# Three float32 layers on one core: the first three tiles' steps written out anew, a second output bank for two tiles, other weight addresses

## What is computed

```python
for t in range(S):      # S = 768, 8 heads of width 64
    state = gamma * state + outer(k[t], v[t])
    x[t] = q[t] @ state / sqrt(64)
h = x @ w_in            # 512 -> 1024
e = exp(h - max(h)); sm = e / (sum(e) + 1e-9); solu = h * sm
ln = (solu - mean(solu)) / sqrt(var(solu) + 1e-6) * g_ln
x = ln @ w_out          # 1024 -> 512
h = x @ w_in2           # 512 -> 2048
y = (h * cos(h)) @ w_out2
```

## Time and profile before

| | us |
|---|---|
| median of 3 runs (958.66 to 959.32) | 958.75 |
| the profiled execution | 958.3 |
| its span | 956.5 |
| PE busy | 931.4 |
| DVE busy | 732.5 |
| ACT busy | 563.0 |
| POOL busy | 265.3 |

### The profile page before, as it was taken

The page is one execution under the profiler, slowest core; times in us unless marked ns, Lnnn a source line. Parts: engine busy times, 40 slices in busy tenths (PEclk is TensorE's granted clock), DMA queues, the critical chain, the costliest instruction groups (busy, mean ns, idle before and its releaser), DMA issues.

```text
span 956.5 us, 14711 instructions
## 1 busy us (share of the span) xinstructions
PE 931.4 (97%) x4992; PEld 826.1 (86%) x4992; DVE 732.5 (77%) x1054; ACT 563.0 (59%) x923; POOL 265.3 (28%) x260
## 2 busy tenths in 40 slices
...
DMA packets 106520, 148.18 MB, mean 155 GB/s; under 512 B 7408, under 2 KB 77040, under 8 KB 106480
## 3 DMA queue, kind: packets, MB, share of 16 engines
...
...
## 4 chain that ended last, share of the span: by engine, by line
PE 81%; DVE 12%; issue 4%; ACT 1%; DMA 1%; POOL 0%; DVEq 0%; SPq 0%; ACTq 0%; POOLq 0%
PE bank L318 26%; PE bank L321 26%; PE bank L320 26%; DVE p_l L1111 2%; DVE q_l L1095 1%; PE bank L620 1%; DVE work L1161 1%; DVE p_m L1104 1%; DVE x_l L1135 1%; DVE nmax L1155 1%; DVE wo_out L1209 1%; PE bank L655 1%; DVE z_l L1189 1%; ACT x_h L788 1%; DVE work L1201 1%
## 5 line engine op out<-in xcount | busy, mean ns | idle before, releaser
L321 PE MATMUL bank<-yc_h,ring 128*128 128x384 f32 x448 | 150.6, 336 | 0.0
L320 PE MATMUL bank<-yc_l,ring 128*128 128x384 f32 x448 | 150.5, 336 | 0.0
L318 PE MATMUL bank<-yc_h,ring 128*128 128x384 f32 x448 | 150.3, 336 | 0.0
L1238 DVE SCALAR_TENSOR_TENSOR gg<-turns,c 128x768 f32<-128x768 int32 x64 | 61.1, 954 | 63.8 <-ACT turns L859 63.8
L1035 POOL TENSOR_TENSOR y_raw<-y_raw,t 128x768 f32<-128x768 f32 x4 | 7.4, 1851 | 362.0 <-DVE yc_l L1220 362.0
L865 ACT ACTIVATE gg<-gg 128x768 f32<-128x768 f32 x64 | 54.2, 847 | 81.0 <-DVE gg L1245 80.9
L859 ACT ACTIVATE turns<-c 128x768 int32<-128x768 f32 x64 | 54.2, 847 | 80.5 <-DVE c L1308 78.0
L318 PEld LDWEIGHTS bank<-yc_h,ring 128*128 128x128 f32 x448 | 84.2, 188 | 8.3 <-issue 0.4
L320 PEld LDWEIGHTS bank<-yc_l,ring 128*128 128x128 f32 x448 | 84.1, 188 | 8.1
L321 PEld LDWEIGHTS bank<-yc_h,ring 128*128 128x128 f32 x448 | 84.1, 188 | 0.0
L318 PE MATMUL bank<-w1i_h,x_h 128*128 128x512 f32 x192 | 78.5, 409 | 5.0 <-DVE x_l L1135 3.6
...
## 6 DMA issues: line engine op xcount, KB each, us to landing
ring<-w_split SPq DMA_DIRECT2D x224, 256.0 KB, 2.8
...
```

The lines of the kernel that those rows point to most:

```text
L318: eng.matmul(dst, ah, bh, start=first and i == 0, stop=False, skip_group_check=read_between)
L320: eng.matmul(dst, ah, bl, start=False, stop=False, skip_group_check=read_between)
L321: m = eng.matmul(dst, al, bh, start=False, stop=last_one and i == n - 1, skip_group_check=read_between)
L1238: dve.scalar_tensor_tensor(gg[:, r, :], turns[:, r, :], -TWO_PI_HI, flat(c_32[:, r, :, :]), ALU.mult, ALU.add)\
```

## The change

- `head` is written out anew. The steps of the first three tiles stand in one explicit list, and `STEP` holds from n = 3 on. Among what moves: on tile 0, PL and ST stand ahead of PK of tile 1, O1 directly behind O0; SC of tile 1 and W1 2 and 3 stand ahead of L1a of tile 0; PK of tile 2 stands behind EX and U of tile 0. W1 0 to 3 stay in front of L1a; W1 4 stands behind SL of tile 1, and units 5, 6 and 7 stand behind SC, T0 and T1 in n = 3 (`between`), so 4 to 7 all come later than before.
- DVE's `nmax` gets a step name of its own, NM. In `STEP` it stands behind L1b, where it was; in the explicit list behind ST of tile 1.
- `bank_o`: O1 of tiles 0 and 1 writes the bank `ps_t`, so it doesn't wait for `x_l` of O0. T0 of tile 0, which writes that bank next, gets a wait for the last `x_l` of tile 1.
- q of tile 0 is scaled by DVE instead of POOL (`q_sc0`), and for the first two tiles DVE starts on the first half of `q_h` (`q_hi0`) before ACT has made the second.
- The memsets are split: four in front (`zeros(0)`), four in DVE's PK of tile 1 (`zeros(1)`), with the semaphore `q_zero` for SC. PE starts on `ld_cst` instead of `setup`.
- Loads: q of tile 0 goes first, then the constants, then k; k and q of tile 1 stand ahead of the first W1 unit.
- `ident` is read where it lies in the constants, so its copy and its tile go. With that and other fillers, `w1i`, `x` and `work` lie 320 bytes higher, `z`, `w1o` 192 bytes lower, `w2o` 576 bytes lower. Within 512 bytes the start of `w1i_h` goes from 224 to 32 and that of `w2o` from 0 to 448.

```diff
-        ("DL", 1), ("T1", 3), ("EX", 2), ("ST", 1), ("WS", 0),
+        ("NM", 2), ("DL", 1), ("T1", 3), ("EX", 2), ("ST", 1), ("WS", 0),
...
-            sb1("to_64_bytes", [128, 4])
+            sb1("to_512_bytes", [128, 84])
-            ident = sb1("ident", [128, 128])
-            sb3("to_w2o", [128, 656])
+            sb3("to_w2o", [128, 512])
+        ident = cst[:, ID0:QSC0]
...
-        early = {(1, "PL"): (0,), (1, "PQ"): (1,), (1, "O1"): (2, 3),
-                 (2, "O0"): (4,), (2, "PN"): (5,), (2, "CEN"): (6, 7)}
...
+        head += [("PK", 0), ("PQ", 0), ("PV", 0), ("PN", 0)]
+        head += [("SC", 0), ("DL", 0), ("PL", 0), ("ST", 0), ("PK", 1), ("O0", 0), ("O1", 0),
+                 ("PQ", 1), ("W1", 0), ("SH", 0), ("PV", 1), ("W1", 1), ("PN", 1), ("SL", 0)]
+        head += [("SC", 1), ("W1", 2), ("W1", 3), ("L1a", 0), ("L1b", 0), ("DL", 1), ("PL", 1),
+                 ("ST", 1), ("NM", 0), ("EX", 0), ("U", 0), ("PK", 2), ("O0", 1), ("O1", 1),
+                 ("SH", 1), ("PQ", 2), ("PV", 2), ("SQ", 0), ("CEN", 0), ("PN", 2), ("VAR", 0),
+                 ("SL", 1), ("W1", 4)]
+        between = {(3, "SC"): 5, (3, "T0"): 6, (3, "T1"): 7}
+        for n in range(3, TILES):
+            for name, behind in STEP:
                 head += [(name, n - behind)] * (n >= behind)
+                if (n, name) in between:
+                    head.append(("W1", between[n, name]))
...
+        def bank_o(t, b, g):
+
+            return ps_t if g == 1 and by_dve(t, b) else ps_o
...
+            sp.dma_start(raw[:, 0, 0, :], qT[0, :, :]).then_inc(ld_kq[0], 16)
             sp.dma_start(cst[:, 0:MASK0], consts[:, 0:MASK0]).then_inc(ld_cst, 16)
-            load_kq(0, 0)
+            sp.dma_start(raw[:, 0, 1, :], kT[0, :, :]).then_inc(ld_kq[0], 16)
...
+            load_kq(1, 1)
             load_w1(0)
-            load_kq(1, 1)
...
                     wait(pe, k_lo, b, t)
+                    if by_dve(t, b):
+                        pe.wait_ge(q_zero, t + 1)
...
-                    wait(pe, xl_done, b, t, 2, g - 1)
+                    if by_dve(t, b):
+                        wait(pe, xl_done, b, t - 1, 2, g)
+                    else:
+                        wait(pe, xl_done, b, t, 2, g - 1)
...
+                        if isinstance(b, int) and t == 0:
+                            wait(pe, xl_done, b, FIRST - 1, 2, 1)
...
-            pe.wait_ge(setup, SETUP)
+            pe.wait_ge(ld_cst, 16)
...
                 if name == "PK" and by_dve(t, b):
+                    if t == 1:
+                        zeros(1)
+                    if t == 0:
+                        q = raw[:, par, 0, :]
+                        loaded(dve, ld_kq, t, b)
+                        dve.tensor_tensor(q, q, qsc, ALU.mult).then_inc(q_sc0, 1)
                     wait(dve, k_hi, b, t)
...
-                    wait(dve, q_hi, b, t)
                     if by_dve(t, b):
+                        wait(dve, q_hi0, b, t)
...
-                elif name == "L1b":
+                elif name == "NM":
                     wait(dve, l1_done, b, t, 2, 1)
```

More of the change, by code:

```diff
@@ L46 @@
 TS = SUPER // 128
-QSC0 = 0
+ID0 = 0
+QSC0 = ID0 + 128
 KSC0 = QSC0 + PAIRS * C
 GC0 = KSC0 + H
-ID0 = GC0 + PAIRS
-MASK0 = ID0 + 128
+MASK0 = GC0 + PAIRS
 NCONST = MASK0 + H * C
@@ L61 @@
 W1_SLOTS = 4
-SETUP = 6
 FIRST = 2
@@ L184, in build @@
         ksc = cst[:, KSC0:GC0]
-        gam_c = cst[:, GC0:ID0]
+        gam_c = cst[:, GC0:MASK0]
+        ident = cst[:, ID0:QSC0]
         e_b, u_b, c_b = work[:, 0, :], work[:, 1, :], work[:, 2, :]
@@ L195, in build @@
         ld_w1 = [sem(f"ld_w1_{u}") for u in range(W1_UNITS)]
-        setup = sem("setup")
+        setup, q_zero = sem("setup"), sem("q_zero")
         w1_hi, w1_lo = sem("w1_hi"), sem("w1_lo")
-        q_sc, n_sc = sem("q_sc"), sem("n_sc")
+        q_sc0, q_sc, n_sc = sem("q_sc0"), sem("q_sc"), sem("n_sc")
+        q_hi0 = sem("q_hi0")
         k_hi, q_hi, n_hi, v_hi = sem("k_hi"), sem("q_hi"), sem("n_hi"), sem("v_hi")
@@ L256, in build @@
         head, tail = [], []
-        for n in range(TILES):
-            first = []
-            if n == 0:
-                first = [("PK", 0), ("PQ", 0), ("PV", 0), ("PN", 0)]
-            elif n == 1:
-                first = [("SC", 1), ("PK", 0), ("PL", 1), ("DL", 1), ("ST", 1), ("O0", 1), ("PV", 0),
-                         ("PQ", 0)]
-            elif n == 2:
-                first = [("PK", 0), ("PV", 0), ("SC", 1)]
-            steps = first + [part for part in STEP if part not in first]
-            for name, behind in steps:
+        head += [("PK", 0), ("PQ", 0), ("PV", 0), ("PN", 0)]
[8 more added lines that the diff above has]
+            for name, behind in STEP:
                 head += [(name, n - behind)] * (n >= behind)
-                head += [("W1", u) for u in early.get((n, name), ())]
+                if (n, name) in between:
+                    head.append(("W1", between[n, name]))
         body = [(name, n - behind) for n in range(TILES) for name, behind in STEP]
@@ L276, in build @@
         tail += [("L1a", last), ("T0", last - 1), ("YH", P6), ("YL", P6), ("YH", P5), ("L1b", last),
-                 ("T1", last - 1), ("EX", last), ("P", P1), ("TBL", 0), ("LA", last - 1),
+                 ("NM", last), ("T1", last - 1), ("EX", last), ("P", P1), ("TBL", 0), ("LA", last - 1),
                  ("U", last), ("CEN", last), ("P", P2), ("SQ", last), ("LB", last - 1),
@@ L590, in step @@
                                           q_of(q_h, par, p), q_of(q_l, par, p)))
-                        m = products(pe, ps_o[:, o], terms, True, True)
+                        m = products(pe, bank_o(t, b, g)[:, o], terms, True, True)
                     m.then_inc(o_done, 1)
@@ L766, in step @@
                 elif name == "PQ":
-                    wait(act, q_sc, b, t)
+                    if isinstance(b, int) and b == 0 and t == 0:
+                        act.wait_ge(q_sc0, 1)
+                    else:
+                        wait(act, q_sc, b, t - 1)
                     for a in range(2):
@@ L771, in step @@
                             "p (c t) -> p c t", c=PAIRS))
+                        if a == 0 and by_dve(t, b):
+                            m.then_inc(q_hi0, 1)
                     m.then_inc(q_hi, 1)
@@ L788, in step @@
                         m = act.copy(x_h[r, par, 2 * g:2 * g + 2, :],
-                                     two_pairs(ps_o[r, :])[:, :, a, :])
+                                     two_pairs(bank_o(t, b, g)[r, :])[:, :, a, :])
                     m.then_inc(xh_done, 1)
```

18 lines of the change are left out of this document (10 added, 8 removed).

## The result

| | before | after |
|---|---|---|
| median, measured side by side (6 runs each) | 959.04 | 965.38 (964.88 to 966.7) |
| ratio, with its interval | | 1.007 (1.0058 to 1.0082) |
| the profiled execution | 958.3 | 964.9 |
| its span | 956.5 | 963.1 |
| PE busy | 931.4 | 932.1 |

The forecast was 968.5 with a range of 961 to 972. The sign and the range held; the time was 3.1 too high. The walk through the filling turned out right to 0.8 us at each of its marks and to 0.4 at 70 us. What was missing is a gain of 2.4 in the third layer that the forecast had put at nothing, and 0.8 that came back when a later PE wait went away.

The account below looks back on a forecast made before the run. PE alone bounds from 50 us; before that, in the filling, DVE makes it wait. The terms 7.0 + 1.6 + 1.1 + 0.5 = 10.2 on 958.3 gave 968.5, range 961 to 972.

Parts of the forecast that it names:

- The walk through the filling: Following DVE's order, with ACT and POOL feeding it, to date PE's groups in the filling; it gave 10.2 us later.
- Part 1: Loads and q of tile 0 on DVE: SC 0 at 9.2 with POOL first, 8.3 undisturbed, instead of 9.7.
- Part 2: SC 1 at 21.3, -0.2: the memsets in PK 1 cost 2.3 and eat the gain.
- Part 3: L1 of tile 0: PE waits 3.1 for w1i_l 2, half clock lasts to 34.5, L1b ends 4.8 later.
- part 4: NM behind ST: L1a of tile 1 at 43.7 after a 3.5 wait, T0 of tile 0 at 49.4, +1.8.
- Part 4's credit for the bank: Second bank credited with 1.7 on the path at O1 of tile 1, and nothing in tile 0.
- Part 5: T1 of tile 0 at 59.4, +7.0, through late POOL and W1 work; then O0 of tile 2 +1.6, clock +1.1 and +0.5.
- Addresses: Moved starts of w1i, w1o and w2o: taken as nothing, bound 2.3 us to each side.
- Rival (c): Addresses count in every 128x512 matmul, 4 ns each, 9 us either way: 959.5 or 977.5; chance 0.04.
- (a): Same chain in the filling, mild: DVE and POOL hardly collide, clock holds; sum 2.5, time 961; chance 0.13.
- (b): New order brings T1 of tile 0 at 52.3 or earlier; priced at -4, time 954; chance 0.10.
- (d): Loads bound the filling, so the change doesn't do what it says; time 958.5; chance 0.05.

Follow-up runs that it names:

- the three parts undone: Changed kernel with memsets in front, NM 0 ahead of ST 1, W1 5, 6, 7 behind T0, T1, O0 in n = 3: 964.73, ratio 1.0063.

## Why the prediction held, and the one term that failed

The marks of the walk, in us of the profiled execution:

| place | forecast | measured |
|---|---|---|
| SC 0 | 9.2 | 9.42 |
| SC 1 | 21.3 | 21.52 |
| third product of L1a 0, behind a wait of | 29.5, 3.1 | 29.69, 2.71 |
| half clock until | 34.5 | 34.0 |
| L1a of tile 1, behind a wait of | 43.7, 3.5 | 43.32, 3.05 |
| its third product | 45.3 | 45.15 |
| T0 of tile 0 | 49.4 | 49.19 |
| T1 of tile 0, behind a wait for `z_l` of | 59.4, 5.5 | 58.64, 4.79 |
| O0 of tile 2 | 61.3 | 60.56 |
| late behind the filling, at 70 us | 10.2 | 9.8 |
| from there to 523 us | 0 | -0.8 |
| third layer | 0 | -2.4 |
| whole, by the span | +10.2 | +6.6 |

**Part 1** took the late end of SC 0, because POOL's scaling of kn might come first. It did, by 0.1: POOL's operation ran at 7.68 to 8.72 and the second half of `q_l`, from 7.76, took 1.51. But POOL was not free near 6.8, as the forecast had it; it had waited for the load of tile 0's v. The undisturbed end was seen too. In the run with NM ahead of ST, whose program up to there is the same, POOL started at 8.14 and both halves of `q_l` took 0.7: SC 0 at 8.62, where the forecast had put 8.3. In the other runs with the new loads and q on DVE it lay between 9.42 and 10.06. Here one row decides nothing: in the profiled executions of programs that are the same up to there (but for addresses), SC 0 lay between 8.62 and 10.06 and SC 1 at 21.38, 21.52, 23.10 and 23.13. The parts undone one by one can't be read closer than that in the timelines. It also means that the marks came out to 0.8 partly by luck: the same walk would have missed SC 1 by 1.8 had another execution been profiled.

**Part 2** said that the memsets eat the gain; with all of them in front SC 1 came at 20.79, 0.7 earlier, not the 2.3 of the walk. (PE idled from 15.8, not from 17 as it says.) The rest went to DVE's collisions with POOL, and nothing of it was left at T1.

**Part 3** (wait for `w1i_l` 2, clock cut in two) and **part 4** (NM behind ST, the third product no longer late) came as told, place by place. For the clock, the forecast had waits of 3 us and more followed by half clock, "as at 35 to 43". The waits in those rows are 1.82, 1.44 and 2.65, so they didn't show it. The new traces do: directly behind the waits of 5.75 and 4.79 of the changed kernel, and of 5.42 and 5.35 at SC 1 in the runs with the addresses of before and with W1 moved, the products stood at half clock; behind the waits of 2.71 and 3.05 they did so some 1.1 us later. For the 5.42:

```profile
23.45 0.42 PE L320 MATMUL bank<-q_l,k_h 128*128 128x256 f32 x1
23.67 0.41 PE L321 MATMUL bank<-q_h,k_l 128*128 128x256 f32 x1
```

They are 0.21 apart, where 0.12 is full clock. (The windows view gives a clock of 1.00 in this stretch of these two runs, whose traces hold no record of the clock before 28.8; the distances decide.) For a shorter wait it isn't settled: one of 1.82 in front of O1 of tile 1 was followed by full clock until 44.6 in the kernel before, and by half clock from 37.7 in the run with `w2o` alone moved.

**Part 4's credit for the bank** was the step that was wrong without showing in the sum. The forecast gave it 1.7 at O1 of tile 1 and nothing in tile 0, "where SC 1 waits for `q_l` anyway". Without the bank the time is 7.9 longer, and SC 1 4.3 later. `q_l` would itself be late then: in DVE's order it stands behind the `x_l` of O1. The walk was made with the bank in place, so its marks were right; only the account of what each part is worth was not. The rule that was weighed there (the Trainium skill, "TensorE: Matmul & The Clock Gate", section "HAM oscillation — how this bites in real kernels", that PSUM double-buffering gave a thin kernel no further gain once its loop kept PE warm) would have the bank worth nothing; in the new order it is worth 7.9. That doesn't contradict it, since its condition, that PE is kept warm, isn't met in this filling, where the clock is at half for part of the time. In the kernel before the clock is at half too for part of the filling (0.21 between products at 21.50 to 24.18), so that all the new parts together were worth less than 1 there is no test of it either.

**Part 5**, the largest term, was right in most of its links: POOL's operations of tile 2 at 41.5 to 50.4, the centring and `s_l` at 2.67, where before they took 0.75 and 0.69 undisturbed, `w1o_l` 4 at 50.91 (forecast 50.2), a DVE idle time of 1.92 for `w1o_h` 5, `z_l` at 57.90 to 58.58 (58.6), T1 6.3 late instead of 7.0. One link was another than told: the forecast let `w1o_l` 4 wait for ACT's `w1o_h` 4, but that was done by 49.4, and DVE itself came 1.5 later, out of the stretched `s_l`. So the collisions with POOL carried more of this term, and ACT's order less. From O0 of tile 2 (7.9 late) to 70 us (9.8) the half clock cost 1.9; the forecast had 1.6 (its own factors, 12 at 0.1 and three at 0.2, give 1.8).

**Addresses** is the term that failed. "I take nothing, with 2.3 us to each side as bound": it was -2.4 by the runs that move addresses alone, just past that bound. The reason given was that `w1i` and `w2o` had different offsets in the kernel before and means of 409 and 391 ns. Those two means differ by the clock of the filling as well, so they could not tell a difference of 6 ns between places; and the bound of 1 ns each had nothing behind it. What the address did is read from two fixed instructions, 2.4, and from the medians of the two runs on the old kernel, 2.4 again; no duration of a single group tells it, since the groups went both ways. The forecast also said that PE has "no slack to give it back" behind the filling. It had 0.8: the wait for `p_l` at 212 us is there in the runs that are up to 8.5 late by then, and gone in all that are 10.3 or more late, but also in one that is 1.4 late (the order of before in the changed kernel), so its cause is left open. Rival (c) had the right mechanism with the wrong reach: it let every 128x512 matmul change, and only those of one tile did (with the 128x384 ones going the other way).

Of the rivals, (a) was refuted by the rows at 45 to 51, where DVE and POOL did collide; (b) by T1 at 58.64; (d) by the run with the order of before. The time lies in the lower half of the range because the address's gain and these 0.8 were taken at nothing.

Why the order loses is shown as far as this: DVE is the engine that ends PE's waits in the filling, and the new order gives it 2.3 of memsets and POOL's collisions where it has no idle time, and then idle times of 5.41 and 1.92 in front of DL 1 and `w1o_h` 5. No single move undone brings it back (0.3 at most by the medians, which is noise), and three together bring T1 back by 5.3 and the time by 0.65. So which move costs the 8.6 isn't shown. One candidate is left untested: W1 2 and 3, whose high parts now stand behind both `p_h` on ACT, with the wait of 2.71 in L1 of tile 0 and a second stretch of half clock behind it. Neither this nor the place of W1 4 and of O0 and O1 of tile 1 was undone alone. Only the whole order was, and it gives 8.6.

## To carry to other kernels

Follow a new order through the engine that ends the waits, with every collision it causes, before judging it by the engine that waits: the walk over DVE, ACT and POOL gave the filling's loss to 0.4 us (closer than one execution is to the next), while repairs at single waits gave next to nothing. A resource that seems idle in the old order (here a second bank) can be what the new one stands on; price it by taking it away in the new order. And a change that moves tiles in SBUF is two changes: run the addresses alone on the old kernel, since a few ns on each of a thousand matmuls came to 2.4 us here, as much as a wait in the filling.

## What the runs showed of the chip

- The start of `w2o` in SBUF changes the time of its products: 388 to 391 ns at 448 within 512 bytes, 391 to 397 at 0 and at 256. With 448 the products of tiles that had not moved took 1 to 3 ns more. The net is 2.4 us of 958.6. The mechanism is open.
- Operations of DVE that took 0.69 alone took 1.2 to 1.8 beside POOL's (`q_l`, `v_l`, `n_l`, `k_l`); the centring took 0.75 alone and 1.65 or 2.67, and `s_l` 0.68, 1.41 or 2.66, by how much of POOL's work fell on them.
- PE idle times of 5.35 to 5.75 in front of SC 1 were followed by half clock each time. The same idle time of 1.82 in front of O1 of tile 1 was followed by full clock until 44.6 in one execution (the kernel before) and by half clock from 37.7 in another (`w2o` alone moved). With the three parts undone the clock came back at 64.5, as in the changed kernel, though PE had begun 4.1 earlier with O0 of tile 2.
- Programs that are the same up to SC 0, but for addresses, put it anywhere from 8.62 to 10.06. Part of that is whether POOL's scaling of kn fell on one half of `q_l`, on the other or on none (8.62); the load of k also landed up to 0.6 apart.
